# Five of a group's twenty fp32 sums, and two later adds, go from VectorE to GpSimd in a Strassen MLP

## The chip, the cores and the metric

One Trainium2 chip, one core of it. The metric is the device time of the whole program in microseconds; the traces are of one execution each.

## The reference

All in fp32. An attention without softmax (`out = q (k^T v)`, RMS-normalised) gives x of 8 x 576 tokens by 512 features. Then two MLPs with residuals follow, both 512 to 2048 to 512:

```python
# first: Fourier mixing and a norm ahead of the MLP
mixed = np.real(np.fft.fft(np.fft.fft(x, axis=1), axis=2))
u = x + mixed
un = (u - mean(u)) / np.sqrt(var(u) + 1e-6)
x2 = u + np.maximum(un @ w_ch1, 0.0) @ w_ch2
# second: a rank-32 mixing over the tokens
u = x2 + (x2.transpose(0, 2, 1) @ U @ V).transpose(0, 2, 1)
out = u + np.maximum(u @ w_ch1b, 0.0) @ w_ch2b
```

## The kernel before

**Stages.** Up to about 265 us of the span the attention and the Fourier transforms run, a batch at a time. All the rest is the two MLPs. The 4608 tokens are worked off in 12 groups g of 768: groups 0 to 5 are the first MLP, groups 6 to 11 (`g >= NS`) the second, over the same tokens.

**Products.** Each matrix product of a group is one level of Strassen's scheme: seven block products instead of eight, on sums and differences of blocks. In the up half (512 to 2048) the moving operands are sums of blocks of the input `a_sb`, in the down half (2048 to 512) sums of blocks of the hidden layer `h_sb`. `SIDE` says which: product 1 takes block 11 + 22, product 4 takes 21 - 11, 3 takes 12 - 22, 7 takes 21 + 22, 6 takes 11 + 12, and products 2 and 5 take one block alone. The down half runs over the products in the order 2, 5, 1, 4, 3, 7, 6 and over four quarters k of the hidden layer each: 28 steps.

**Splitting.** A step needs its 128 x 768 operand as two fp32r parts. For a product with two blocks there are three instructions, on three tiles of a ring of five entries: the sum `t_raw` (VectorE, `raw_dn`, L1358), its rounded part `t_hi` (ScalarE, `hi_dn`, L1073), and the rest `t_lo` = `t_raw` - `t_hi` (VectorE, `lo_dn`, L1339). TensorE then runs 12 matmuls (hi x hi, lo x hi, hi x lo, twice two; L832 to L834 in the up half, L849 to L851 in the down half). In the up half it is GpSimd that makes the sums (`raw`, L1569).

**Order.** Every engine has its order written out by hand: loops over g and over 56 steps t (28 up, 28 down), in which an engine issues what stands at its t. Entry n of the down half is used by TensorE at t = n + 28; the sum is issued at t = n + 24, `t_hi` at n + 25, `t_lo` at n + 26. `t_raw` of n waits for two things: that TensorE is through with the entry five before it in the ring (`entry_room`: the step before loop step n + 24 has ended) and that the hidden blocks are final (`blocks_final`). An engine takes its instructions strictly in the order issued.

VectorE further reads the results of the down half out of PSUM (`read`: d5 at t = 36, d1 at t = 40, d7 at t = 52, d6 at t = 56; in groups 6 to 11 also d4 at t = 44 and d3 at t = 48, which ScalarE does in groups 0 to 5). In groups 6 to 11 `add_first` (L1411, VectorE, t = 46 and 50) adds what d1 has left in `ch_sb` to the input blocks 11 and 22; both wait for d1, and d7 and d6 wait for both (`v_ready`).

In groups 0 and 6, the first of each MLP, the weights come unsplit: GpSimd sums pairs of weight blocks (`sum_slot`, L1559, at t = 20 to 30 and 40, 42, 44, 46, each behind its DMA), ScalarE rounds them (L981) and VectorE makes the rest (`split_slot_lo`, L1271). GpSimd otherwise has the up-half sums (at t = 5, 12, 52, 54, 55) and, in groups 1 to 4, the sums of the second MLP's weights.

Of the kernel before, what the change touches and what calls it, by code (L numbers as in the profile page):

```python
# [23 lines left out]
NS = NTILE // 2  # L24
NG = 2 * NS
NCH = 2 * CH
# [82 lines left out]
def dve_count(g, name, k=0):  # L109
    return sum(len(dve_events(x)) for x in range(g)) + [e[1:] for e in dve_events(g)].index((name, k)) + 1  # L110
# [45 lines left out]
def in_load_at(g):  # L156

    t = in_at(g)[1] // 2 * 2
    return t, t + 2


def build_program(nc, k_main, k_rest, v_main, v_rest, q_t, g_norm, wr1a, wr2a, wr1b, wr2b, u_perm, v_perm,
# [3 lines left out]
    ALU = mybir.AluOpType  # L166
# [90 lines left out]
    def a_block(g, name):  # L257
        a, b = int(name[0]) - 1, int(name[1]) - 1
        return a_sb[g % 2 if g >= NS else 0][:, 2 * a:2 * a + 2, TILE * b:TILE * (b + 1)]
# [4 lines left out]
    def ch_block(name):  # L264
        a, b = int(name[0]) - 1, int(name[1]) - 1
        return ch_sb[:, 2 * a:2 * a + 2, TILE * b:TILE * (b + 1)]
# [10 lines left out]
    with ExitStack() as ctx:  # L277
# [85 lines left out]
        def raw_made(g, e):  # L363

            pool = dve = 0
            for x in range(NENT * g + e + 1):
                gx, ex = divmod(x, NENT)
                if ex < len(UP_ENTRIES):
                    pool += len(SIDE[UP_ENTRIES[ex]]) > 1
                else:  # L370
                    dve += len(SIDE[DN_STEPS[ex - len(UP_ENTRIES)][0]]) > 1
            return pool, dve

        def sides(g, e):
# [536 lines left out]
        def _(act):  # L911
# [151 lines left out]
            def hi_dn(g, n):  # L1063
                i, k = DN_STEPS[n]
                e = len(UP_ENTRIES) + n
                r = (NENT * g + e) % ENT_RING
                if len(SIDE[i]) == 1:
                    act.wait_ge(step, entry_room(g, e))
                    act.wait_ge(act_read, act_count(g, "r" + SIDE[i][0], k))
                    nc.scalar.activation(t_hi[r][:, :, :], h_block(SIDE[i][0], k), ACT.Copy).then_inc(hi_ready, 1)  # L1070
                else:
                    act.wait_ge(raw_dve, raw_made(g, e)[1])
                    nc.scalar.activation(t_hi[r][:, :, :], t_raw[r][:, :, :], ACT.Copy).then_inc(hi_ready, 1)  # L1073

            def read(g, name, k):
# [120 lines left out]
        def _(dve):  # L1196
# [152 lines left out]

            def raw_dn(g, n):  # L1350
                i, k = DN_STEPS[n]
                if len(SIDE[i]) == 1:
                    return
                e = len(UP_ENTRIES) + n
                dve.wait_ge(step, entry_room(g, e))
                dve.wait_ge(act_read, blocks_final(g, e))
                x, y, op = sides(g, e)
                nc.vector.tensor_tensor(t_raw[(NENT * g + e) % ENT_RING][:, :, :], x, y, op).then_inc(raw_dve, 1)  # L1358

            def read(g, name, k):  # L1360
# [34 lines left out]
                else:  # L1395
# [8 lines left out]
                        if g > NS:  # L1404
                            dve.wait_ge(out_stored[block], 16 * (g - NS))
                    nc.vector.tensor_tensor(ch_block(block), both(DN_PAIR[i]), added, ALU.add).then_inc(dve_read, 1)

            def add_first(g, block):

                dve.wait_ge(dve_read, dve_count(g, "d1"))  # L1410
                nc.vector.tensor_tensor(a_block(g, block), a_block(g, block), ch_block("22"), ALU.add).then_inc(v_ready, 1)  # L1411

            def add_residual(g, j):
                n = NCH * g + j
# [31 lines left out]
            for g in range(NG):  # L1446
                more = g < NG - 1
                for t in range(NSTEP):
                    if g and t == 0:
                        read(g - 1, "d6", 0)  # L1450
                    if t == 0:
                        lo_up(g, 2)
                    if t == 2:
                        lo_up(g, 3)
                    if t == 3:
                        lo_up(g, 4)
                    for at, name, k in dve_events(g):
                        if at == t:
                            read(g, name, k)
                    if t == 8:  # L1460
                        lo_up(g, 5)
                    if t == 15:
                        lo_up(g, 6)
                    if t in (21, 22, 27, 28):
                        lo_dn(g, (21, 22, 27, 28).index(t))
                    if 29 <= t < 33:
                        lo_dn(g, t - 25)
                    if 34 <= t < 54:
                        lo_dn(g, t - 26)
                    if 32 <= t < 52:  # L1470
                        raw_dn(g, t - 24)
                    if g >= NS and t == 46:
                        add_first(g, "11")
                    if g >= NS and t == 50:
                        add_first(g, "22")
                    if more and t == 54:
                        lo_up(g + 1, 0)
                    if more and t == 55:
                        lo_up(g + 1, 1)
                    if g == 0 and t == 2:  # L1480
                        fix_row(B - 1)
                    if g == 0 and t == 36:
                        nc.vector.memset(up_raw[:, :, :], 0.0).then_inc(up_zeroed, 1)
                    if g == 0 and t == 43:
                        dve.wait_ge(up_split_hi, 1)
                        nc.vector.tensor_tensor(up_lo[:, :, :], up_raw[:, :, :], up_hi[:, :, :].bitcast(F32),
                                                ALU.subtract).then_inc(up_split_lo, 1)
                    if g == NS - 1 and t == 0:
                        dve.wait_ge(p_stored["v"], 32 * 8)
                        nc.vector.memset(vp_raw[:, :, :], 0.0).then_inc(vp_zeroed, 1)  # L1490
                    if g == NS - 1 and t == 9:
                        dve.wait_ge(vp_split_hi, 1)
                        nc.vector.tensor_tensor(vp_lo[:, :, :], vp_raw[:, :, :], vp_hi[:, :, :].bitcast(F32),
                                                ALU.subtract).then_inc(vp_split_lo, 1)
                    if 1 <= g <= NS:
                        if t - 1 in OUT_AT:
                            add_residual(g - 1, OUT_AT.index(t - 1))
                        if t - 3 in OUT_AT:
                            split_x2_lo(g - 1, OUT_AT.index(t - 3))
                        for P in range(4):  # L1500
                            n = 9 * P + 8
                            if n // NCH == g - 1 and t - 2 == GATHER_AT[n % NCH]:
                                turn_gathered(P)
                    if more:
                        if g + 1 < NS:
                            if t in LN_AT:
                                statistics(3 * (g + 1) + LN_AT.index(t))
                            if t - 2 in LN_AT:
                                layer_norm(3 * (g + 1) + LN_AT.index(t - 2))
                        elif t - 1 in mix_at(g):  # L1510
                            add_mixed(NCH * (g + 1) + mix_at(g).index(t - 1))
                    if (g, t - 8) in UNIT_AT:
                        split_unit_lo(UNIT_AT[g, t - 8])
                    for n in RAW_SLOTS:
                        if NSTEP * g + t == max(0, 2 * n - 6):
                            split_slot_lo(n)
# [3 lines left out]
        def _(pool):  # L1520
# [39 lines left out]

            def raw(g, e):
                r = (NENT * g + e) % ENT_RING
                pool.wait_ge(a_ready, NCH * (g + 1))
                if entry_room(g, e):
                    pool.wait_ge(step, entry_room(g, e))
                else:
                    stored_before(pool, e)
                x, y, op = sides(g, e)
                nc.gpsimd.tensor_tensor(t_raw[r][:, :, :], x, y, op).then_inc(raw_pool, 1)  # L1569

            for g in range(NT):
                weigh(0, g)
# [17 lines left out]
            for g in range(NG):  # L1590
                more = g < NG - 1
                for t in range(NSTEP):
                    if t == 5:
                        raw(g, 5)
                    if t == 12:
                        raw(g, 6)
                    if more and t == 52:
                        raw(g + 1, 0)
                    if more and t == 54:
                        raw(g + 1, 2)  # L1600
                    if more and t == 55:
                        raw(g + 1, 3)
                    if (g, t - 4) in UNIT_AT:
                        sum_unit(UNIT_AT[g, t - 4])
                    for n in RAW_SLOTS:
                        if NSTEP * g + t == 2 * n - 8 and summed_slot(n):
                            sum_slot(n)
# [74 lines left out]
```

## Time and profile before

| | us |
|---|---|
| median of 3 runs | 1824.33 |
| lowest and highest | 1823.0, 1835.87 |
| the profiled execution | 1823.0 |
| its span | 1820.9 |

The times are of the whole program; the span is that of the profiled execution's trace, from its first instruction to its last, and every row below counts from the span's start. PE is TensorE, DVE VectorE, ACT ScalarE, POOL GpSimd. An instruction's duration in the trace holds the time that it stood still for a memory port, so the same instruction with longer and shorter durations tells of something beside it. VectorE's instructions overlap by about 0.08 us, since one starts before the one ahead is written out.

### The profile page before, as it was taken

How to read it: one execution, taken by the hardware profiler on the slowest of the kernel's cores; microseconds unless marked ns; L12 is line 12 of the kernel's file. 1: busy time of each engine (PE TensorE's matmuls, PEld its weight loads, DVE VectorE, ACT ScalarE, POOL GpSimd, SP SyncE). 2: the span in 40 equal slices, each digit the busy share in tenths (PEclk: the TensorE clock that was granted, in tenths of full speed). 3: DMA queues.
4: the chain of work that ended last, by engine and by line, in shares of the span. 5: the costliest groups of instructions: out<-in, count | busy, mean ns of one | idle time of the engine just before them, and what ended most of it. 6: DMA issues, size and time to landing. Idle time of an engine off the chain costs nothing.

```text
span 1820.9 us, 25843 instructions
## 1 busy us (share of the span) xinstructions
PE 1738.5 (95%) x9908; PEld 1673.3 (92%) x9908; DVE 1374.4 (75%) x1631; ACT 786.0 (43%) x1126; POOL 432.9 (24%) x356
## 2 busy tenths in 40 slices
PE   6889879989999999999999999899999999999999
PEld 5667769979999999999999999799999999999999
DVE  5779987997777877867866858965956857758567
ACT  2333344554444544445444436434334434444442
POOL 2889973331120120120110013220110100100200
PEclk9889989999999999999999999999999999999999
DMA  8487557988787887887876778876766766767663
GB/s 256 161 272 250 201 201 282 370 332 283 262 303 261 283 287 258 289 286 247 297 260 232 257 246 310 333 275 231 251 236 237 257 234 242 255 231 254 224 249 128
DMA packets 123820, 470.04 MB, mean 258 GB/s; under 512 B 12274, under 2 KB 49650, under 8 KB 84019
## 3 DMA queue, kind: packets, MB, share of 16 engines
q1 hardware_dynamic: 122482, 467.21, 73.4%
q8 instruction: 81, 1.33, 0.3%
q10 hardware_dynamic: 1216, 1.18, 0.2%
q14 instruction: 41, 0.33, 0.0%
HBM read 389.70 MB, written 78.64 MB: 257 GB/s over the span
## 4 chain that ended last, share of the span: by engine, by line
PE 80%; DVE 12%; issue 3%; POOL 3%; DMA 2%; SPq 1%; ACT 0%; DVEq 0%; POOLq 0%; ACTq 0%
PE pair L832 12%; PE pair L834 12%; PE pair L833 12%; PE pair L849 12%; PE pair L851 12%; PE pair L850 12%; DVE t_lo L1339 2%; PE tr_ps L716 2%; PE pair L623 2%; DVE t_raw L1358 2%; DMA in_sb<-x_dram 1%; DVE w_sb L1271 1%; DMA v_sb<-v_rest 1%; DVE eo_sb L1229 1%; POOL x_sb L1528 1%
## 5 line engine op out<-in xcount | busy, mean ns | idle before, releaser
L849 PE MATMUL pair<-t_hi,w_sb 128*128 128x384 f32 x1344 | 460.4, 343 | 17.1 <-DVE t_lo L1339 16.7
L832 PE MATMUL pair<-t_hi,w_sb 128*128 128x384 f32 x1344 | 459.8, 342 | 7.0 <-DVE h_sb L1376 6.9
L851 PE MATMUL pair<-t_hi,w_sb 128*128 128x384 f32 x1344 | 456.9, 340 | 0.0
L850 PE MATMUL pair<-t_lo,w_sb 128*128 128x384 f32 x1344 | 456.8, 340 | 0.0
L833 PE MATMUL pair<-t_lo,w_sb 128*128 128x384 f32 x1344 | 455.1, 339 | 0.0
L834 PE MATMUL pair<-t_hi,w_sb 128*128 128x384 f32 x1344 | 455.0, 339 | 0.0
L1569 POOL TENSOR_TENSOR t_raw<-a_sb 128x768 f32<-128x768 f32 x60 | 126.1, 2103 | 920.1 <-PE pair L851 636.6
L1073 ACT ACTIVATE t_hi<-t_raw 128x768 fp32r<-128x768 f32 x240 | 202.6, 847 | 287.6 <-DVE t_raw L1358 287.6
L1339 DVE TENSOR_TENSOR t_lo<-t_raw,t_hi 128x768 fp32r<-128x768 f32 x300 | 306.7, 1028 | 12.9 <-ACT t_hi L1061 9.2
L849 PEld LDWEIGHTS pair<-t_hi,w_sb 128*128 128x128 f32 x1344 | 253.5, 189 | 23.8 <-DVE t_lo L1339 23.6
L832 PEld LDWEIGHTS pair<-t_hi,w_sb 128*128 128x128 f32 x1344 | 252.2, 188 | 14.3 <-issue 9.0
L1358 DVE TENSOR_TENSOR t_raw<-h_sb 128x768 f32<-128x768 f32 x240 | 241.1, 1005 | 23.4 <-PE pair L851 22.9
L833 PEld LDWEIGHTS pair<-t_lo,w_sb 128*128 128x128 f32 x1344 | 252.4, 188 | 3.1
L850 PEld LDWEIGHTS pair<-t_lo,w_sb 128*128 128x128 f32 x1344 | 253.6, 189 | 0.3
L851 PEld LDWEIGHTS pair<-t_hi,w_sb 128*128 128x128 f32 x1344 | 253.4, 189 | 0.0
L834 PEld LDWEIGHTS pair<-t_hi,w_sb 128*128 128x128 f32 x1344 | 252.2, 188 | 0.0
L1339 DVE TENSOR_TENSOR t_lo<-h_sb,t_hi 128x768 fp32r<-128x768 f32 x96 | 98.5, 1038 | 23.4 <-ACT t_hi L1070 23.4
L1380 DVE TENSOR_TENSOR h_sb<-pair,h_sb 128x768 f32<-128x768 f32 x48 | 46.0, 958 | 84.3 <-PE pair L834 84.2
L1271 DVE TENSOR_TENSOR w_sb<-w_raw,w_sb 128x1024 fp32r<-128x1024 f32 x76 | 105.1, 1383 | 2.4 <-ACT w_sb L981 2.3
L1528 POOL TENSOR_TENSOR x_sb<-x_sb,gn_sb 96x256 f32<-96x256 f32 x96 | 84.2, 908 | 57.7 <-DVE x_sb L1213 57.4
L1371 DVE TENSOR_TENSOR h_sb<-pair,h_sb 128x768 f32<-128x768 f32 x48 | 46.0, 958 | 65.9 <-PE pair L834 65.9
L1070 ACT ACTIVATE t_hi<-h_sb 128x768 fp32r<-128x768 f32 x96 | 78.7, 842 | 36.0 <-PE pair L851 32.6
(148 smaller groups left out, 2005.3 us busy)
## 6 DMA issues: line engine op xcount, KB each, us to landing
w_sb<-wc SPq DMA_DIRECT2D x260, 1024.0 KB, 4.9
wc<-w_sb SPq DMA_DIRECT2D x28, 1024.0 KB, 5.7
w_raw<-wr1a SPq DMA_DIRECT2D x24, 512.0 KB, 5.1
w_raw<-wr1b SPq DMA_DIRECT2D x24, 512.0 KB, 4.3
wc<-pb SPq DMA_DIRECT2D x16, 640.0 KB, 4.8
w_raw<-wr2a SPq DMA_DIRECT2D x10, 1024.0 KB, 7.0
wc<-pb_v SPq DMA_DIRECT2D x16, 640.0 KB, 5.7
w_raw<-wr2b SPq DMA_DIRECT2D x10, 1024.0 KB, 7.2
```

Source lines behind the costliest of these rows:

```text
L832: nc.tensor.matmul(ps, w_hi, hi[:, x, :], start=(fresh and x == 0), stop=False, skip_group_check=True)
L833: nc.tensor.matmul(ps, w_hi, lo[:, x, :], start=False, stop=False, skip_group_check=True)
L834: last = nc.tensor.matmul(ps, w_lo, hi[:, x, :], start=False, stop=(x == 1), skip_group_check=True)
L849: nc.tensor.matmul(ps, w_hi, hi[:, f, :], start=(fresh and k == 0 and f == 0), stop=False, skip_group_check=True)
L850: nc.tensor.matmul(ps, w_hi, lo[:, f, :], start=False, stop=False, skip_group_check=True)
L851: last = nc.tensor.matmul(ps, w_lo, hi[:, f, :], start=False, stop=(k == 3 and f == 1), skip_group_check=True)
L1073: nc.scalar.activation(t_hi[r][:, :, :], t_raw[r][:, :, :], ACT.Copy).then_inc(hi_ready, 1)
L1271: nc.vector.tensor_tensor(w_sb[r][:, 1, :, :, :], w_raw[r][:, 1, :, :, :], w_sb[r][:, 0, :, :, :].bitcast(F32), ALU.subtract).then_inc(w_l ...
L1339: nc.vector.tensor_tensor(t_lo[r][:, :, :], src, t_hi[r][:, :, :].bitcast(F32), ALU.subtract).then_inc(lo_ready, 1)
L1358: nc.vector.tensor_tensor(t_raw[(NENT * g + e) % ENT_RING][:, :, :], x, y, op).then_inc(raw_dve, 1)
L1528: last = nc.gpsimd.tensor_tensor(x, x, gn_sb[:, :].unsqueeze(1).to_broadcast([PT, H // 2, HD]), ALU.mult)
L1569: nc.gpsimd.tensor_tensor(t_raw[r][:, :, :], x, y, op).then_inc(raw_pool, 1)
```

## The change

The sum `t_raw` of every down-half entry with k = 3 is made by GpSimd instead of VectorE, where it is a sum of two blocks (products 1, 4, 3, 7, 6; loop steps t = 35, 39, 43, 47, 51). ScalarE waits for GpSimd's counter for these. Both `add_first` of groups 6 to 11 go to GpSimd too, to t = 41, behind each other. Within a loop step GpSimd issues the new instructions ahead of a weight sum of the same step. Nothing is left out or computed otherwise.

```diff
+POOL_KS = (3,)
+
+
+def by_pool(i, k):
+    return k in POOL_KS
@@ raw_made
-                    dve += len(SIDE[DN_STEPS[ex - len(UP_ENTRIES)][0]]) > 1
+                    i, k = DN_STEPS[ex - len(UP_ENTRIES)]
+                    if len(SIDE[i]) > 1:
+                        pool, dve = (pool + 1, dve) if by_pool(i, k) else (pool, dve + 1)
@@ scalar: hi_dn
-                    act.wait_ge(raw_dve, raw_made(g, e)[1])
+                    if by_pool(i, k):
+                        act.wait_ge(raw_pool, raw_made(g, e)[0])
+                    else:
+                        act.wait_ge(raw_dve, raw_made(g, e)[1])
@@ vector: raw_dn
-                if len(SIDE[i]) == 1:
+                if len(SIDE[i]) == 1 or by_pool(i, k):
                     return
@@ vector: add_first and its two calls
-            def add_first(g, block):
-
-                dve.wait_ge(dve_read, dve_count(g, "d1"))
-                nc.vector.tensor_tensor(a_block(g, block), a_block(g, block), ch_block("22"), ALU.add).then_inc(v_ready, 1)
...
-                    if g >= NS and t == 46:
-                        add_first(g, "11")
-                    if g >= NS and t == 50:
-                        add_first(g, "22")
@@ gpsimd: raw
-                pool.wait_ge(a_ready, NCH * (g + 1))
-                if entry_room(g, e):
+                if e < len(UP_ENTRIES):
+                    pool.wait_ge(a_ready, NCH * (g + 1))
+                    if entry_room(g, e):
+                        pool.wait_ge(step, entry_room(g, e))
+                    else:
+                        stored_before(pool, e)
+                else:
                     pool.wait_ge(step, entry_room(g, e))
-                else:
-                    stored_before(pool, e)
+                    pool.wait_ge(act_read, blocks_final(g, e))
                 x, y, op = sides(g, e)
                 nc.gpsimd.tensor_tensor(t_raw[r][:, :, :], x, y, op).then_inc(raw_pool, 1)
+
+            def raw_dn(g, n):
+                i, k = DN_STEPS[n]
+                if len(SIDE[i]) > 1 and by_pool(i, k):
+                    raw(g, len(UP_ENTRIES) + n)
+
+            def add_first(g, block):
+
+                pool.wait_ge(dve_read, dve_count(g, "d1"))
+                nc.gpsimd.tensor_tensor(a_block(g, block), a_block(g, block), ch_block("22"), ALU.add).then_inc(v_ready, 1)
@@ gpsimd: the loop over t
+                    if 32 <= t < 52:
+                        raw_dn(g, t - 24)
+                    if g >= NS and t == 41:
+                        add_first(g, "11")
+                        add_first(g, "22")
```

## Rows read from the trace of the kernel before

**Rows 1.** The page: its head, and busy time, share and instructions by engine.

```profile
span 1820.9 us, 25843 instructions
PE 1738.5 (95%) x9908; PEld 1673.3 (92%) x9908; DVE 1374.4 (75%) x1631; ACT 786.0 (43%) x1126; POOL 432.9 (24%) x356
```

**Rows 2.** Busy time of each engine in groups 0, 6 and 8.

```profile
core 0: us, PE busy (x) PEld busy (x) DVE busy (x) ACT busy (x) POOL busy (x), PEclk, DMA share, GB/s
285.00:404.00 119.00, 107.65 (x595) 103.88 (x594) 110.20 (x114) 60.92 (x77) 40.47 (x14) 0.99 0.93 345
...
1047.00:1191.00 144.00, 134.08 (x740) 128.21 (x740) 118.17 (x119) 69.30 (x87) 39.71 (x15) 0.98 0.84 303
...
1319.00:1445.00 126.00, 124.64 (x712) 123.63 (x711) 86.59 (x94) 52.86 (x66) 10.78 (x6) 1.00 0.70 242
```

**Rows 3.** TensorE's waits for `t_lo`: whole span, 280 to 410, 1080 to 1200.

```profile
PE pair L849 <- DVE t_lo L1339: 16.7, 16, 2.7
...
PE pair L849 <- DVE t_lo L1339: 8.6, 7, 2.2
...
PE pair L849 <- DVE t_lo L1339: 8.2, 9, 2.7
```

**Rows 4.** Busy time in finer stretches of groups 0, 6 and 8, columns as [rows 2].

```profile
355.00:395.00 40.00, 31.46 (x159) 28.90 (x158) 40.00 (x36) 17.86 (x22) 13.53 (x5) 0.96 0.92 336
1147.00:1197.00 50.00, 41.70 (x209) 38.08 (x208) 50.00 (x43) 20.20 (x24) 21.77 (x7) 0.93 0.88 328
1397.00:1437.00 40.00, 40.00 (x228) 40.00 (x228) 35.96 (x42) 15.79 (x19) 0.00 (x0) 1.00 0.75 253
```

**Rows 5.** Groups by line (busy, mean), and line L1569's durations (min/median/max, ns).

```profile
L1358 DVE TENSOR_TENSOR t_raw<-h_sb 128x768 f32<-128x768 f32 x240 | 241.1, 1005 | 23.4 <-PE pair L851 22.9
L1073 ACT ACTIVATE t_hi<-t_raw 128x768 fp32r<-128x768 f32 x240 | 202.6, 847 | 287.6 <-DVE t_raw L1358 287.6
...
L1569 POOL TENSOR_TENSOR t_raw<-a_sb x60: 1807/1855/4334, 260.0 to 1723.6; 128x768 f32<-128x768 f32 x60
```

**Rows 6.** Timeline of group 8: start, duration; VectorE, and starts of TensorE's steps.

```profile
1413.10 0.96 DVE L1388 TENSOR_TENSOR ch_sb<-pair,ch_sb 128x768 f32<-128x768 f32 x1 [0.57 <-PE pair L851]
1413.97 0.95 DVE L1339 TENSOR_TENSOR t_lo<-t_raw,t_hi 128x768 fp32r<-128x768 f32 x1
1414.84 0.95 DVE L1358 TENSOR_TENSOR t_raw<-h_sb 128x768 f32<-128x768 f32 x1
...
1417.45 0.95 DVE L1339 TENSOR_TENSOR t_lo<-t_raw,t_hi 128x768 fp32r<-128x768 f32 x1
...
1420.05 0.95 DVE L1358 TENSOR_TENSOR t_raw<-h_sb 128x768 f32<-128x768 f32 x1
1421.58 0.96 DVE L1394 TENSOR_TENSOR ch_sb<-pair,a_sb 128x768 f32<-128x768 f32 x1 [0.57 <-PE pair L851]
...
1419.26 0.34 PE L849 MATMUL pair<-t_hi,w_sb 128*128 128x384 f32 x1
...
1421.38 0.34 PE L849 MATMUL pair<-t_hi,w_sb 128*128 128x384 f32 x1
```

**Rows 7.** Timeline where GpSimd and VectorE run side by side: groups 8 and 0.

```profile
1438.65 2.10 POOL L1569 TENSOR_TENSOR t_raw<-a_sb 128x768 f32<-128x768 f32 x1 [86.11 <-PE pair L851]
1438.96 0.95 DVE L1406 TENSOR_TENSOR ch_sb<-pair,a_sb 128x768 f32<-128x768 f32 x1
1439.83 1.74 DVE L1339 TENSOR_TENSOR t_lo<-t_raw,t_hi 128x768 fp32r<-128x768 f32 x1
...
1442.89 2.12 POOL L1569 TENSOR_TENSOR t_raw<-a_sb 128x768 f32<-128x768 f32 x1 [2.14 <-PE pair L851]
1443.23 2.60 DVE L1339 TENSOR_TENSOR t_lo<-a_sb,t_hi 128x768 fp32r<-128x768 f32 x1
...
332.80 6.29 POOL L1559 TENSOR_TENSOR w_raw<-w_raw 128x1024 f32<-128x1024 f32 x1 [4.78 <-DMA w_raw<-wr2a]
...
361.42 2.75 POOL L1559 TENSOR_TENSOR w_raw<-w_raw 128x1024 f32<-128x1024 f32 x1 [2.90 <-DMA w_raw<-wr2a]
361.87 3.12 DVE L1358 TENSOR_TENSOR t_raw<-h_sb 128x768 f32<-128x768 f32 x1
```

## The prediction

> **What bounds the kernel now.** I read the page first: TensorE is busy for 95% of the span, VectorE for 75%, GpSimd for 24% [rows 1]. That looks like a kernel bound by TensorE with a VectorE in reserve, but a share over the whole span hides stages. So the windows by group came next [rows 2]: group 8 is an ordinary one, TensorE is full and VectorE has 39 of 126 us left, while groups 0 and 6 (where weights are still being summed and split) have VectorE at 110 of 119 and 118 of 144 us, and TensorE short. The waits of TensorE [rows 3] name one wait of the second phase that matters: 16.7 us for `t_lo` of L1339, 16 times. All 16 lie in groups 0 and 6. The finer windows [rows 4] show how much that is in all. In 40 undisturbed us of group 8 TensorE starts 228 matmuls, one every 0.175 us; in 355 to 395 us it starts 159, so 69 x 0.175 = 12 us are lost; in the 50 us from 1147 it starts 209 where 285 fit, 13 us lost. In both stretches VectorE is busy for every microsecond. The granted clock is 0.96 and 0.93 there and 1.00 in group 8. So some 25 us hang on VectorE's queue, and the rest of the second phase hangs on TensorE.
>
> **What is removed.** Five `t_raw` of each group (the last quarter, k = 3, of products 1, 4, 3, 7, 6) leave VectorE: 60 in all; in groups 6 to 11 the two `add_first` leave too: 12. Back to back, VectorE starts such an instruction every 0.87 us (1413.97, 1414.84 [rows 6]). So VectorE is freed of 60 x 0.87 + 12 x 0.87 = 63 us. In the ordinary groups this is worth nothing by itself, since TensorE doesn't wait for VectorE there. In groups 0 and 6 it would be 5 x 0.87 = 4.4 and 7 x 0.87 = 6.1 us.
>
> **What is added.** The same 72 instructions on GpSimd. VectorE's `t_raw` is 1.00 us on average; the nearest rows on GpSimd are its own `t_raw` of the same size, 1.86 us in the median of 60, up to 4.33 [rows 5]. 72 x 1.85 = 133 us more on an engine busy for 433 of 1821: there is room. The price is elsewhere. What happens when both engines work on SBUF is in [rows 7]. In group 8 GpSimd's `t_raw` starts at 1438.65; VectorE's L1406, which reads PSUM and one SBUF operand, takes its usual 0.95 us beside it; the `t_lo` after it, with two SBUF operands, takes 1.74 instead of 0.95. The `t_lo` at 1443.23 behind another GpSimd `t_raw` takes 2.60, and the `t_raw` at 361.87 behind a GpSimd weight sum 3.12. The excess ends each time with the GpSimd instruction: VectorE doesn't slow down, it stands still. The other way round GpSimd stands still too: its weight sum at 332.80 took 6.29 us, the same one at 361.42 only 2.75.
>
> So a moved instruction gives VectorE 0.87 and takes back 0.79 (1.74 - 0.95, when a PSUM read covers half of it) to 1.65 (2.60 - 0.95): net -0.08 to +0.78 us for each, if VectorE is busy at the time; nothing if GpSimd falls into a gap. The Trainium skill (SBUF — State Buffer, "Who interferes with whom") says the same of a VectorE instruction with two SBUF inputs and a GpSimd one that reads SBUF: whichever gets the pair first holds it for the whole instruction, the other blocks fully. By that rule alone, every one of the 72 meeting a busy VectorE would cost the upper figure; the trace agrees on the standing still, but shows GpSimd also passed over (6.29 us), which is what gives the lower figure.
>
> **Where the moved ones fall.** The raw at loop step t may start when step t-1 has ended. They are at t = 35, 39, 43, 47, 51, and VectorE's next item is always a read of PSUM at t+1 (36, 40, 44, 48, 52; in groups 0 to 5 those of 44 and 48 are ScalarE's). In group 8 VectorE has a gap there: it waits 0.57 us for the read at 1413.10 and for that at 1421.58 [rows 6], 1.4 us once the raw before is gone. GpSimd's 1.85 us then lies in the gap and under the PSUM read. So the 35, 39, 47, 51 of the ordinary groups cost nothing. For the `t_lo` that follows, GpSimd has two loop steps of time (12 x 0.175 = 2.1 us each) against 1.85 + 0.85 on ScalarE [rows 5]: no wait. If that cover is gone, it costs 0.78 each.
>
> *Groups 7 to 11, the adds.* They are the dear part. Both wait for d1, whose sum ends at 1414.05, and stand in GpSimd's queue ahead of the raw of t = 43. VectorE works without a pause from 1413.10 to 1421.00 here. If GpSimd gets in after each VectorE instruction, the two adds and the raw (allowed at 1419.26, the start of step 43) block three VectorE instructions, 3 x 1.65 = 4.95 us, before the `t_lo` that ends at 1417.45 + 0.95 = 1418.40. TensorE needs that at 1421.38 (step 44): 2.98 us to spare, so it waits 2.0 us. If GpSimd is held off until the gap after 1420, the adds run at about 1420.1 and 1422.0, the raw of 43 ends near 1426.4, ScalarE's part and the `t_lo` near 1428.2, and step 47 (start 1421.38 + 3 x 2.12 = 1427.7) waits 0.5. A wait costs more than itself: 25 us were lost for 16.7 us of waits in 16, of which some 5 are half clock (0.04 x 40 + 0.07 x 50), so 0.2 us each; say 0.3. That is 0.8 to 2.3 us for each of five groups, 4 to 11.5. Both orders occur in [rows 7], so I take the middle, 7.5.
>
> *Group 0.* VectorE has no gap. Five raws x (-0.08 to +0.78) = -0.4 to 3.9 us. GpSimd gets in at once as often as not, and the sums in its queue make alternation likelier; I take 2.5. The raw of t = 43 stands behind the sum of t = 42, which waits for its weights' DMA ([rows 7]: 2.90 us idle before 361.42); it is still needed only two loop steps later by a VectorE that is late itself, so no price.
>
> *Group 6.* Seven x (-0.08 to +0.78) = -0.6 to 5.5 us. The adds stand between the weight sums here; three GpSimd instructions more in a stretch where the sums already block; I take 4.5.
>
> *Clock.* A longer stall can lengthen the half-clock stretch that it brings, now 0.07 x 50 = 3.5 us in group 6: 0 to 5 us, I take 1.5. *Groups 1 to 5* have no adds and, as group 8, no wait for `t_lo` [rows 3]; should one blocked `t_lo` become late there, that is 0.78 + 0.3, so 0 to 1 us; I take 0.
>
> Sum: 7.5 + 2.5 + 4.5 + 1.5 = 16 us on the profiled execution's own 1823.0 us (span 1820.9 plus 2.1 around it), which is 1.3 below the median shown: **1839 us**. Bounds from the ends: 4 - 0.4 - 0.6 = +3 to 11.5 + 3.9 + 5.5 + 5 + 1 = +27.
>
> **Rivals.** *Relief* (the other side, if too little for the 1%): in groups 0 and 6 GpSimd slips its work wholly under PSUM reads and waits, VectorE is 10.5 us shorter there and TensorE follows, and the adds find gaps: 1823 - 10.5 = 1812. For it: VectorE is the cause of the 25 us. Against: in groups 0 and 6 there is no gap to slip into [rows 4]. It decides once the mean block of a moved instruction is below the 0.87 us that moving it frees. *Nothing moves*: GpSimd is held off and gets in only under PSUM reads, -0.08 each, the adds cost the lower end: 1823 + 3 = 1826. For it: the 6.29 us sum. *Full alternation*: every moved instruction blocks 1.65 and stalls bring clock: 1823 + 27 = 1850, with some more if groups 1 to 5 begin to stall as well.
>
> **How the numbers follow.** Forecast 0.50, nothing moves 0.17, full alternation 0.22, relief 0.11. Range: 1816 to 1855. A measurement of this kernel tells about 1% from no change, 18 us: faster than 1806 needs more than relief gives: 0.04. Slower than 1842.6 holds the rival of full alternation and the upper third of the forecast: 0.36. Within 1%: 0.60.
>
> **What would show it.** `t_lo` and `t_raw` of VectorE get a longer mean though there are 60 fewer of them; GpSimd's `t_raw` and `add_first` show 2.1 to 2.6 us, some over 4. TensorE's wait for `t_lo` rises above 16.7 us and has new entries in groups 7 to 11, one or two a group near steps 44 to 47. Wrong would be: no wait there (the adds found room), or fewer than 12 and 13 us lost in groups 0 and 6 (relief), or a wait for GpSimd on ScalarE that reaches TensorE (then the queue order, not the blocking, sets the price).

## The result and the profile after

| | before | changed |
|---|---|---|
| median, 8 runs each, us | 1832.2 | 1849.01 |
| lowest and highest | 1823.0, 1835.87 | 1840.04, 1852.56 |
| the profiled execution | 1823.0 | 1847.24 |
| its span | 1820.9 | 1844.9 |

The ratio is 1.0101, with an interval of 1.0079 to 1.0124: the changed kernel is slower by about 18.5 us. The ratio rests on more runs than the table's eight (25 of the changed kernel, with a median of 1849.86), whose medians alone are 16.8 us apart. The two profiled executions are 24.2 us apart. Single executions differ by more than the effect: in the twelve traces of this case group 0 begins between 263.6 and 278.6 us, though no kernel changes anything ahead of it. So amounts for a whole kernel go by ratios, and amounts of a stretch by the lengths of the groups below.

The page of the changed kernel, its head, the engines and the groups by line (busy, mean in ns, idle time before them and its releaser); the last line is of the full list of groups:

```profile
span 1844.9 us, 25843 instructions
PE 1744.3 (95%) x9908; PEld 1677.4 (91%) x9908; DVE 1376.6 (75%) x1559; ACT 784.6 (43%) x1126; POOL 612.4 (33%) x428
...
L1351 DVE TENSOR_TENSOR t_lo<-t_raw,t_hi 128x768 fp32r<-128x768 f32 x300 | 345.4, 1158 | 13.5 <-ACT t_hi L1070 10.0
L1576 POOL TENSOR_TENSOR t_raw<-h_sb 128x768 f32<-128x768 f32 x60 | 152.0, 2534 | 575.5 <-PE pair L860 575.5
...
L1370 DVE TENSOR_TENSOR t_raw<-h_sb 128x768 f32<-128x768 f32 x180 | 207.6, 1154 | 19.8 <-PE pair L860 19.8
...
L1586 POOL TENSOR_TENSOR a_sb<-a_sb,ch_sb 128x768 f32<-128x768 f32 x12 | 30.0, 2522 | 5.6 <-DVE ch_sb L1400 5.6
```

VectorE executes 72 instructions fewer than in [rows 1] (1559 against 1631) and is busy 2.2 us longer (1376.6 against 1374.4). The 63 us that were to be freed are all there again, as longer durations: its `t_raw` takes 1154 ns on average instead of the 1005 of [rows 5]. The 60 moved sums take GpSimd 2.53 us each and the 12 moved adds 2.52, where the prediction had 1.85 for the instruction alone. The busy share of VectorE, 75% on both pages, tells nothing of this; instructions and means do.

TensorE's waits for `t_lo` in the changed kernel: whole span, group 0 (280 to 414 us), group 6 with its neighbours (1060 to 1215), and the rest (1215 to 1845). The columns are the sum in us, the number, and the longest:

```profile
PE pair L858 <- DVE t_lo L1351: 34.2, 24, 5.5
...
PE pair L858 <- DVE t_lo L1351: 12.5, 7, 3.4
...
PE pair L858 <- DVE t_lo L1351: 13.7, 7, 5.5
...
PE pair L858 <- DVE t_lo L1351: 8.0, 10, 1.0
```

Against [rows 3] the waits of groups 0 and 6 grew from 8.6 and 8.2 to 12.5 and 13.7, and the last line is new: ten waits in groups 7 to 11, two of them in group 8.

How long each group takes, from its first matmul to the next group's (in us, from the traces; "t32" is the part of groups 0 and 6 from step 32 on, in which all moved instructions lie; g7-10 is a mean of four; e1 to e10 are the experiments below; groups 1 to 3 take 129.0 to 129.2 in all of them but e9, where they take 133.7, and group 5 takes 130.9 in all):

```
                           g0     g0 t32  g4     g6     g6 t32  g7-10  g11
before                     137.3  63.6    129.1  146.5  66.4    125.6  118.8
changed                    145.1  68.3    129.4  150.8  71.1    127.7  120.9
e1 sums only               143.3  64.7    129.5  147.4  67.4    125.7  118.8
e2 adds only               141.6  63.5    129.0  147.2  67.2    126.5  119.6
e3 adds at t = 46, 50      141.0  64.6    129.4  150.5  70.5    128.5  119.2
e4 late weight sums, DVE   134.3  60.3    129.1  143.1  63.0    125.6  118.8
e5 idle adds               138.3  63.8    129.1  145.9  66.3    129.1  120.3
e6 idle fills              137.6  63.2    129.1  145.6  65.8    125.8  118.8
e7 sums, not in g0, g6     136.9  63.2    129.4  148.1  66.3    125.7  118.8
e8 all weight sums, DVE    134.4  61.3    129.0  145.3  64.3    125.7  118.8
e9 two quarters            144.7  71.1    133.6  153.6  73.9    130.4  121.5
e10 changed, e4's edit     137.8  63.0    129.5  146.8  66.8    127.8  120.9
```

Where nothing in them differs, groups 1 to 5 and 7 to 11 repeat to 0.3 us, so one trace is enough to read them. Groups 0 and 6 do not: group 0 took 136.9, 137.3, 137.6, 138.3 and 141.6 in the five traces in which nothing in it differs. But that spread lies ahead of t = 32: from there on the same five took 63.2 to 63.8, and group 6 took 65.8 to 66.4 in the four in which nothing in it differs. So for these two groups the columns t32 are the ones to compare. In the changed kernel's group 0, 3.1 of the 7.8 us more were lost before t = 32, ahead of any moved sum, and 4.7 behind it.

### The profile page after: what moved, and what is told of

The parts are those of the page before. It is cut to its first block, busy times and chain, and to the rows that moved or that the text cites. A ratio compares the mean times of both kernels' runs of the same rounds, so it can differ in the third digit from the quotient of the medians.

```text
span 1844.9 us, 25843 instructions
## 1 busy us (share of the span) xinstructions
PE 1744.3 (95%) x9908; PEld 1677.4 (91%) x9908; DVE 1376.6 (75%) x1559; ACT 784.6 (43%) x1126; POOL 612.4 (33%) x428
## 4 chain that ended last, share of the span: by engine, by line
PE 75%; DVE 12%; issue 4%; POOL 4%; DMA 3%; ACT 1%; SPq 1%; DVEq 0%; POOLq 0%; ACTq 0%
PE pair L841 11%; PE pair L843 11%; PE pair L842 11%; PE pair L858 11%; PE pair L860 11%; PE pair L859 11%; DVE t_raw L1370 2%; DVE t_lo L1351 2%; PE tr_ps L725 2%; PE pair L632 2%; DMA in_sb<-x_dram 1%; PE pair L653 1%; DVE w_sb L1283 1%; POOL t_raw L1576 1%; DVE eo_sb L1241 1%
## 5 line engine op out<-in xcount | busy, mean ns | idle before, releaser
L1351 DVE TENSOR_TENSOR t_lo<-t_raw,t_hi 128x768 fp32r<-128x768 f32 x300 | 345.4, 1158 | 13.5 <-ACT t_hi L1070 10.0
L1576 POOL TENSOR_TENSOR t_raw<-h_sb 128x768 f32<-128x768 f32 x60 | 152.0, 2534 | 575.5 <-PE pair L860 575.5
L1370 DVE TENSOR_TENSOR t_raw<-h_sb 128x768 f32<-128x768 f32 x180 | 207.6, 1154 | 19.8 <-PE pair L860 19.8
L1283 DVE TENSOR_TENSOR w_sb<-w_raw,w_sb 128x1024 fp32r<-128x1024 f32 x76 | 109.9, 1446 | 4.3 <-ACT w_sb L990 4.3
L1351 DVE TENSOR_TENSOR t_lo<-h_sb,t_hi 128x768 fp32r<-128x768 f32 x96 | 93.8, 989 | 23.4 <-ACT t_hi L1079 23.4
L1383 DVE TENSOR_TENSOR h_sb<-pair,h_sb 128x768 f32<-128x768 f32 x48 | 46.0, 958 | 65.8 <-PE pair L843 65.8
```

Source lines behind the costliest of these rows:

```text
L1283: nc.vector.tensor_tensor(w_sb[r][:, 1, :, :, :], w_raw[r][:, 1, :, :, :], w_sb[r][:, 0, :, :, :].bitcast(F32), ALU.subtract).then_inc(w_l ...
L1351: nc.vector.tensor_tensor(t_lo[r][:, :, :], src, t_hi[r][:, :, :].bitcast(F32), ALU.subtract).then_inc(lo_ready, 1)
```

## The experiments

The numbers in the expectations are against the kernel before, unless they say otherwise. Theory, as it stood on both traces: every GpSimd instruction that reads SBUF blocks a whole VectorE instruction with two SBUF operands, and the time is lost where a `t_lo` has less slack than the blocks that pile up ahead of it. Rival: GpSimd's longer queue (late sums, weight sums held up behind the new instructions) sets the price.

### e1 and e2: each half of the change alone

e1 keeps the moved sums and takes the adds back to VectorE:

```diff
@@ vector, t = 46 and 50
+                    if g >= NS and t == 46:
+                        add_first(g, "11")
+                    if g >= NS and t == 50:
+                        add_first(g, "22")
@@ gpsimd, t = 41
-                        add_first(g, "11")
-                        add_first(g, "22")
```

> The five sums a group (k = 3) are on GpSimd as in the changed kernel; both adds are back on VectorE at t = 46 and 50. Theory (GpSimd and VectorE exclude each other; only pile-ups behind which TensorE has no slack cost time): groups 7 to 11 keep their old length of 125.7 us, since each sum falls in the gap ahead of a PSUM read, so 10 us of the changed kernel's loss are gone; groups 0 and 6 keep theirs, some 4 to 8 us together: 0.2 to 0.5% slower than before. Rival (the sums are dear wherever they are, by their longer chain over GpSimd): groups 7 to 11 still have 127.7 us each and the whole is 0.8% slower or more.

Measured: 1834.67 against 1828.0, ratio 1.0045 (1.0026 to 1.0063), 8.2 us. Groups 7 to 11 are as before to 0.1 us. The one trace shows less than the ratio: from t = 32 on groups 0 and 6 are 1.0 us longer each, and all groups together, leaving out what comes before t = 32 in these two, less than 3 us, below the 4.8 us at which the interval of the ratio begins.

e2 keeps the moved adds and takes the sums back:

```diff
-POOL_KS = (3,)
+POOL_KS = ()
```

> Only the two adds of groups 6 to 11 are on GpSimd at t = 41; all sums stay on VectorE. Theory: in groups 7 to 11 two blocks of 1.65 us meet 2.98 us of slack at step 44, so TensorE waits 0.3 us where it waited 1.7 to 2.0 with the third block by the sum of t = 43: 0.3 to 0.6 us a group, group 0 unchanged, group 6 0 to 3 us longer: 0.1 to 0.3% slower. Rival (the adds alone carry the 2.1 us a group): groups 7 to 11 at 127.7 us, 0.6% slower or more.

Measured: 1832.72, ratio 1.0023 (1.001 to 1.0036), 4.2 us, and 0.85 a group in groups 7 to 11 (5 x 0.85 = 4.2). That is above the 0.3 to 0.6 expected: two adds block 2 x 1.65 = 3.3 us ahead of the `t_lo` of step 43, which had 2.6 us to spare where the expectation counted with the 2.98 of step 44, and TensorE starts step 43 0.76 us late.

The halves give 8.2 + 4.2 = 12.4 of 18.5 us. The rest is their product: in groups 7 to 11 adds alone cost 0.85 a group, sums alone 0.1, both together 2.1, since the sum of t = 43 is then a third block, ahead of the `t_lo` of step 44. Group 6 from t = 32 on shows the same: 1.0 for the sums, 0.8 for the adds, 4.7 for both.

### e7: the sums, but not in groups 0 and 6

```diff
-def by_pool(i, k):
-    return k in POOL_KS
+def by_pool(g, i, k):
+    return k in POOL_KS and g % NS > 0
@@ the adds back on VectorE, as in e1
```

> The five sums a group go to GpSimd in groups 1 to 5 and 7 to 11 only, 50 in all; in groups 0 and 6 and for the adds all is as before. Theory (a GpSimd sum is free where VectorE has gaps or TensorE has slack): same as before within 0.1%, at most 0.4 us in group 4. Rival: the 0.45% of all sums on GpSimd is spread evenly, so 50 of 60 still cost 0.35% or more.

Measured: 1826.81 against 1828.82, ratio 0.9995 (0.997 to 1.002). 50 sums moved in ordinary groups cost nothing that can be measured; so e1's 8.2 us (4.8 to 11.5 by its interval) would come mostly or wholly from the ten sums of groups 0 and 6, about 0.8 us for each. In the traces the five sums of group 0 cost 1.0 us in e1 and in e3 and 4.7 in the changed kernel, with the same instructions each time. So a moved sum costs something there, between 0.2 and 0.9 us, and no run fixes it closer.

### e5 and e6: is it the reading, or the queue?

Both leave the kernel before as it is and add GpSimd instructions on a tile that nobody uses, at the changed kernel's places (two at t = 41 behind d1, one at t = 43). In e5 they are additions, in e6 fills, which write the same tile and read nothing:

```diff
+                    if g > NS and t == 30:
+                        extra(g, t)
+                    if g > NS and t == 41:
+                        extra(g, t)
+                        extra(g, t)
+                    if g > NS and t == 43:
+                        extra(g, t)
@@ extra, at t = 41 and 43 (at t = 30 a fill in both)
+                # e5
+                nc.gpsimd.tensor_tensor(idle_sb, idle_sb, idle_sb, ALU.add)
+                # e6
+                nc.gpsimd.memset(idle_sb, 0.0)
```

> The kernel before with all its work where it was, and in groups 7 to 11 three extra fp32 additions on GpSimd over a tile of 128x768 that nothing else reads: two at t = 41 behind d1, one at t = 43 (a fill of the tile at t = 30 too). No engine waits for them. Theory (exclusion alone makes the loss): each stops VectorE for 1.65 us, VectorE is freed of nothing, and TensorE loses 2.0 to 2.5 us at steps 42 to 44 of each of these groups: 127.7 to 128.2 us instead of 125.7; group 11 alike. Rival (the loss comes from waiting for GpSimd's late results, its queue or its latency): nobody waits for these results, so the groups stay at 125.7.

> As the run with idle additions, but the extra GpSimd instructions only fill the tile (they write 128x768 and read nothing). Theory (it is the reading of SBUF on both sides that excludes): VectorE's instructions beside them keep 0.95 us and the groups 125.7 us. Rival (any GpSimd access to SBUF stops VectorE): instructions beside a fill are longer by up to its duration.

Measured, one execution each: e5 1847.99, e6 1833.32, beside a median of 1828.82 before. What counts is group 7 to 9: 128.4 us in e5 (2.8 above before), 125.8 or less in e6. (Group 10 of e5 took 131.2, with a half-clock stretch of 3.4 us in it: TensorE's granted clock was at its lower level, 1.2 GHz.) The timeline of group 8 (start, duration, both in us) in e5:

```profile
1427.31 2.23 DVE L1360 TENSOR_TENSOR t_raw<-h_sb 128x768 f32<-128x768 f32 x1
1429.45 2.22 DVE L1341 TENSOR_TENSOR t_lo<-t_raw,t_hi 128x768 fp32r<-128x768 f32 x1
...
1426.60 4.25 POOL L1586 TENSOR_TENSOR idle_sb<-idle_sb 128x768 f32<-128x768 f32 x2 [21.47 <-DVE ch_sb L1390]
```

and in e6:

```profile
1423.99 0.95 DVE L1341 TENSOR_TENSOR t_lo<-t_raw,t_hi 128x768 fp32r<-128x768 f32 x1
1424.85 0.95 DVE L1360 TENSOR_TENSOR t_raw<-h_sb 128x768 f32<-128x768 f32 x1
1425.72 0.95 DVE L1341 TENSOR_TENSOR t_lo<-t_raw,t_hi 128x768 fp32r<-128x768 f32 x1
...
1424.13 1.60 POOL L1586 MEMSET idle_sb<- 128x768 f32 x2 [21.45 <-DVE ch_sb L1390]
```

Nothing waits for these instructions, so no data arrives late and no sum is delayed by a queue; yet e5 alone reproduces the loss of groups 7 to 9, and a bit more than the 127.7 to 128.2 expected; that VectorE keeps its own sums and adds would explain it, but wasn't tested. Fills beside the same VectorE instructions leave each at 0.95. A fill is also shorter (0.80 us against 2.1), so e6 alone would leave duration as an explanation; but VectorE's three instructions beside the fills show no lengthening at all. For groups 7 to 11 this settles it against the queue: the price is what GpSimd's additions do to VectorE's instructions. What an addition has and a fill lacks is the reading of SBUF, so by these two runs it is the reading, not the writing, that collides.

### e3: the adds on GpSimd, but apart

```diff
@@ gpsimd
-                    if g >= NS and t == 41:
-                        add_first(g, "11")
-                        add_first(g, "22")
+                    if g >= NS and t == 46:
+                        add_first(g, "11")
+                    if g >= NS and t == 50:
+                        add_first(g, "22")
```

> The changed kernel with its two adds still on GpSimd, but at t = 46 and t = 50, where VectorE had them. Theory (it is three GpSimd instructions in a row behind d1 that cost): apart, each blocks 1.65 us against at least 2 us of slack, groups 7 to 11 are back at 125.7 us, and 4 to 8 us of groups 0 and 6 stay: 0.2 to 0.5% slower than before. Rival (what VectorE stands still in all decides): the same number of instructions blocks the same time, groups 7 to 11 stay near 127.7 us and the whole at 1% slower.

Measured: 1854.99, ratio 1.0154 (1.0105 to 1.0203): not faster than the changed kernel (1.0101), as the theory had it. Whether it is slower isn't clear, since the intervals overlap. The timeline of group 8 shows what the expectation had overlooked (GpSimd's rows, two of VectorE's, and the TensorE step that waits):

```profile
1440.11 2.33 POOL L1576 TENSOR_TENSOR t_raw<-h_sb 128x768 f32<-128x768 f32 x1 [6.15 <-PE pair L860]
1442.41 1.85 POOL L1586 TENSOR_TENSOR a_sb<-a_sb,ch_sb 128x768 f32<-128x768 f32 x1
1448.59 2.54 POOL L1576 TENSOR_TENSOR t_raw<-h_sb 128x768 f32<-128x768 f32 x1 [4.33 <-PE pair L860]
1451.08 2.58 POOL L1586 TENSOR_TENSOR a_sb<-a_sb,ch_sb 128x768 f32<-128x768 f32 x1
1457.07 2.57 POOL L1576 TENSOR_TENSOR t_raw<-h_sb 128x768 f32<-128x768 f32 x1 [3.41 <-PE pair L860]
1459.60 2.54 POOL L1576 TENSOR_TENSOR t_raw<-a_sb 128x768 f32<-128x768 f32 x1
...
1457.87 2.59 DVE L1370 TENSOR_TENSOR t_raw<-h_sb 128x768 f32<-128x768 f32 x1
1460.38 2.58 DVE L1351 TENSOR_TENSOR t_lo<-t_raw,t_hi 128x768 fp32r<-128x768 f32 x1
...
1463.02 0.44 PE L858 MATMUL pair<-t_hi,w_sb 128*128 128x384 f32 x1 [1.79 <-DVE t_lo L1351]
```

A loop step fixes only the order in the queue. d1 is long done at t = 46, so each add runs directly behind the sum ahead of it: two pairs of blocks instead of one triple, and they lie late in the stretch, just ahead of the sums of t = 51 and 52. From its read of t = 44 to the `t_lo` of step 53 VectorE is blocked 1.06 + 1.65 + 0.80 + 1.65 + 1.65 = 6.8 us and freed of three instructions (both adds and the sum of t = 47), 2.6 us; the `t_lo` of step 53 had 2.3 us to spare before. 2.3 + 2.6 - 6.8 = -1.9, and TensorE waits 1.79. So the quantity that decides is the sum of blocks since VectorE last ran ahead, less what it was freed of, against the slack of the step. In the trace groups 7 to 11 are 12 us longer than before, 3.2 of them with half-clock stretches of 3.4 us in groups 9 and 10 (129.3 us each against 127.7 in 7 and 8); from t = 32 on group 6 is 4.1 us longer and group 0 1.0. That is 17 of the ratio's 28 us (19 to 37 by its interval, over four runs); the other 11 are open.

### e9: a second quarter of the sums on GpSimd

```diff
 def by_pool(i, k):
-    return k in POOL_KS
+    return k in (1, 3)
@@ the adds back on VectorE, as in e1
```

> As the run with the five sums a group on GpSimd and the adds on VectorE (0.45% slower than before), but with the sums of k = 1 there too: ten a group, 120 in all. Theory (each costs its block less the 0.87 us freed where VectorE has no gap): groups 0 and 6 lose twice the 8 us; group 4, where the slack is already used up, 1 us; groups 7 to 11 had 0.3 to 0.7 us left near steps 53 and 54, and lose up to 1 us each: 17 to 24 us, 0.9 to 1.3% slower. Rival (freeing VectorE catches up once enough is moved, since it has 104 us less to do): not slower than the 0.45% of half as many.

Measured: 1893.46 against 1835.06, ratio 1.0314 (1.029 to 1.0339), 58 us, far above the 0.9 to 1.3% expected. Doubling the moved sums costs seven times e1's 8.2 us. Busy time of each engine in the last 40 us of group 2 and of group 5, both of the first MLP (columns as [rows 2]), in e9:

```profile
650.00:690.00 40.00, 37.34 (x204) 35.71 (x205) 39.28 (x29) 17.25 (x23) 21.52 (x10) 1.00 0.78 285
1048.30:1088.30 40.00, 40.00 (x229) 39.87 (x228) 39.96 (x29) 18.08 (x23) 23.82 (x11) 1.00 0.71 261
```

and in the last 40 us of group 2 and of group 5 of the kernel before:

```profile
620.00:660.00 40.00, 40.00 (x228) 40.00 (x227) 36.10 (x38) 19.28 (x23) 5.66 (x3) 1.00 0.88 310
1009.00:1049.00 40.00, 40.00 (x229) 39.87 (x229) 34.40 (x36) 17.86 (x22) 5.57 (x3) 1.00 0.74 262
```

In group 2 VectorE executes 29 instructions instead of 38 and is yet busy for 39.3 instead of 36.1 us (1.35 us for each instead of 0.95), and TensorE starts 204 matmuls instead of 228. Groups 1 to 4, where e7's single quarter was free (0.3 us in group 4), lose 4.6 us each, 0.9 us for each of the second five sums. Group 5 has ten moved sums too and loses nothing: it had less for VectorE to do before (34.4 us), and though VectorE is now busy for all of the 40 us, TensorE starts its 229 matmuls as before. So the price is convex: nothing while gaps and slack take the blocks, and then about what a block takes less what the move frees (0.78 us), or somewhat more.

### e4, e8 and e10: the other way round

If GpSimd's reading is dear in groups 0 and 6, it must pay to take reading off GpSimd there. e4 is the kernel before with the last four weight sums of groups 0 and 6 (slots 24 to 27, the late ones) on VectorE, rounding and rest one loop step later:

```diff
+def by_dve(n):
+    return n % NSLOT >= 24
@@ vector
+                        if NSTEP * g + t == 2 * n - 7 and summed_slot(n) and by_dve(n):
+                            sum_slot(n)      # on nc.vector
@@ gpsimd
-                        if NSTEP * g + t == 2 * n - 8 and summed_slot(n):
+                        if NSTEP * g + t == 2 * n - 8 and summed_slot(n) and not by_dve(n):
```

> The kernel before, with the last four weight sums of group 0 and of group 6 (slots 24 to 27) taken from GpSimd and given to VectorE, each one loop step later, and their two halves of the splitting a loop step later too. Theory (exclusion): VectorE does such a sum in about 1.15 us, and stands still 2.2 us for GpSimd's; each of the two groups gets 4 x 1.05 = 4 us shorter, with some half-clock time less, 6 to 12 us in all, 0.3 to 0.7% faster than before, though VectorE, the late engine there, gets 9 us more work. Rival (VectorE's own work decides): 9 us slower.

Measured: 1819.62 against 1828.0, ratio 0.9956 (0.9941 to 0.9972), 8 us faster. In the trace, the group of the moved sums, one of them in group 0, and TensorE's waits for `t_lo` over the whole span:

```profile
L1276 DVE TENSOR_TENSOR w_raw<-w_raw 128x1024 f32<-128x1024 f32 x8 | 9.7, 1214 | 0.0
...
363.40 1.22 DVE L1276 TENSOR_TENSOR w_raw<-w_raw 128x1024 f32<-128x1024 f32 x1
...
PE pair L853 <- DVE t_lo L1349: 11.3, 12, 2.5
```

The engine that was the bound of these groups got eight instructions of 1.21 us more, and the waits for it fell from 16.7 to 11.3 us. From t = 32 on both groups are 3.4 us shorter. A rival is that the weight sums merely come earlier. It doesn't hold: in the kernel before VectorE waits for nothing from 335 to 404 and from 1130 to 1197 us (the list of its waits is empty there), so sums that come earlier could not by themselves have made it faster; its own instructions had to get shorter. This version beats both kernels.

e8 gives VectorE all twenty weight sums (`by_dve` returns True):

> The kernel before with all 20 weight sums of groups 0 and 6 on VectorE, each one loop step later (the run with 8 of them there was 0.44% faster). Theory (exclusion): the twelve early ones stand in a stretch where VectorE still has gaps, so they give less: 0.5 to 0.8% faster than before, 0 to 6 us better than 8 alone. Rival (VectorE's total work in these groups now decides): 12 x 1.15 = 14 us more of it, slower than the run with 8, near the time of before.

Measured: 1822.66 against 1828.82, ratio 0.9966 (0.9946 to 0.9986). Not better than e4: the theory's further gain did not come. The early sums lie at t = 20 to 30; from t = 32 on groups 0 and 6 take 61.3 and 64.3 us against 60.3 and 63.0 in e4. Why the further sums give nothing, no run shows.

e10 is the changed kernel with e4's edit, so that no late weight sum stands in GpSimd's queue with the moved ones:

> The changed kernel with the last four weight sums of groups 0 and 6 on VectorE, which alone made the kernel before 0.44% faster. Theory: in groups 0 and 6 four blocks of 2.2 us go for 4 x 1.15 us of own work, as before, and groups 7 to 11 stay at 127.7 us: 0.4 to 0.65% slower than before. Rival (GpSimd's queue held by weight sums was what made the moved sums dear in groups 0 and 6): with the queue free these groups lose nothing more by the moved sums, and only the 10 us of groups 7 to 11 less 8 us are left: 0.1% slower.

Measured: 1846.62 against 1835.06, ratio 1.0056 (1.0023 to 1.0088). The gain over the changed kernel's 1.0101 is 0.45%, what e4's edit gave by itself (0.44%), though both intervals leave room for a difference of some 0.3%. Were the weight sums held up behind the moved instructions the main cause, freeing them would have given back more than it gives without the change. For a part the rival stays open: from t = 32 on the edit shortens groups 0 and 6 of the changed kernel by 5.3 and 4.3 us, and of the kernel before by 3.4 each, though single traces of the sums in group 0 differ by as much (e1, e3 and the changed kernel, above). A moved sum can be late without a weight sum in its queue: in group 0 of e10 the two sums from t = 43 on took GpSimd 12.73 us together, and VectorE then stood idle 2.61 us for the first. Groups 7 to 11 stay at 127.8 and 120.9.

## Why the prediction was right, and where it was short

The forecast was +16 us (a ratio of 1.0088), the measured ratio 1.0101 (+18.5 us), inside the range. The predicted 1839 lies 10 us under the changed kernel's median, of which 9.2 us are the base: the kernel before is 1832.2 in eight runs, not the 1823.0 of its profiled execution. The sign and the mechanism held; by the chances, though, "within 1%" had 0.60 and the ratio came out on its edge, 1.01% with an interval over both sides.

| term | forecast | the changed kernel's trace |
|---|---|---|
| groups 7 to 11 | 7.5 (0.8 to 2.3 a group) | 10.5 (2.1 a group) |
| group 0, from t = 32 on | 2.5 | 4.7 (1.0 in e1 and e3) |
| group 6, from t = 32 on | 4.5 | 4.7 |
| clock | 1.5 | within the two above |
| groups 1 to 5 | 0 (0 to 1) | 0.3 (group 4) |
| sum | 16 | 20.2; 18.5 by the ratio |

**The adds of groups 7 to 11, right but mis-sized.** The prediction had two orders and took their middle. The chip takes one of them, in all five groups: GpSimd gets in behind each VectorE instruction. The timeline of group 8 of the changed kernel, VectorE and then GpSimd:

```profile
1428.49 0.96 DVE L1400 TENSOR_TENSOR ch_sb<-pair,ch_sb 128x768 f32<-128x768 f32 x1 [1.44 <-PE pair L860]
1429.36 0.95 DVE L1351 TENSOR_TENSOR t_lo<-t_raw,t_hi 128x768 fp32r<-128x768 f32 x1
1430.23 2.60 DVE L1370 TENSOR_TENSOR t_raw<-h_sb 128x768 f32<-128x768 f32 x1
1432.75 2.60 DVE L1351 TENSOR_TENSOR t_lo<-t_raw,t_hi 128x768 fp32r<-128x768 f32 x1
1435.27 2.59 DVE L1370 TENSOR_TENSOR t_raw<-h_sb 128x768 f32<-128x768 f32 x1
1437.79 0.94 DVE L1351 TENSOR_TENSOR t_lo<-t_raw,t_hi 128x768 fp32r<-128x768 f32 x1
...
1429.53 5.01 POOL L1586 TENSOR_TENSOR a_sb<-a_sb,ch_sb 128x768 f32<-128x768 f32 x2 [0.77 <-DVE ch_sb L1400]
1434.89 2.16 POOL L1576 TENSOR_TENSOR t_raw<-h_sb 128x768 f32<-128x768 f32 x1 [0.36 <-PE pair L860]
```

The three 2.60s are the three blocks of 1.65 and the last `t_lo` is the one that the prediction had at 1418.40 in [rows 6]. The gap ahead of d1 is 1.44 us, as forecast from 0.57. Steps 42 and 43 then take 2.88 and 3.38 us instead of 2.12, together 2.0 us more, what the upper branch had for its wait. It comes in two parts, since two blocks already make the `t_lo` of step 43 late; TensorE's waits between 1400 and 1500 are these two:

```profile
PE pair L858 <- DVE t_lo L1351: 1.6, 2, 1.0
```

The failed part is the choice "both orders occur, so I take the middle": 7.5 us where the upper order alone gives 11.5 and 10.5 were measured. The Trainium skill's rule that the prediction weighed (SBUF — State Buffer, "Who interferes with whom") is what happened here: each blocked instruction stood still until the GpSimd one had ended, 2.60 us beside 0.95.

**The other sums of ordinary groups cost nothing.** The forecast holds: e7 and e1 leave groups 7 to 11 at 125.7 (before 125.6) and groups 1 to 4 within 0.4 us.

**Groups 0 and 6.** The changed kernel's trace has 4.7 + 4.7 = 9.4 us where the prediction had 2.5 + 4.5 + 1.5 = 8.5. That this is so near is partly luck: with the same instructions group 0 lost only 1.0 us in e1 and e3, so 2.5 is a right order of size and no more. In group 6 the adds are dear beside the sums (1.0 and 0.8 alone, 4.7 together), as the prediction's higher figure for it had it. Of the clock: from t = 32 on the kernel before has half-clock stretches (granted clock at the lower level of 1.2 GHz) of 3.4 us in group 0 and 6.8 in group 6, the changed kernel two of 3.4 in group 0 and 6.8 + 3.4 in group 6. One stretch of 3.4 us more in each is, by estimate, worth at most half its length, 1.7 us. (The 3.5 us that the prediction calls the stretch of group 6 is what the stretch of 6.8 us costs at half speed.) What stays unexplained is e1's ratio: 8.2 us for the sums alone, of which its trace shows less than 3.

**A late result of GpSimd in group 0: overlooked.** The prediction gave GpSimd's sum two loop steps, found them enough, and counted its being passed over as VectorE's gain (-0.08). The timeline of group 0 of the changed kernel, where GpSimd's row is the sum of t = 47:

```profile
388.00 7.43 POOL L1576 TENSOR_TENSOR t_raw<-h_sb 128x768 f32<-128x768 f32 x1 [6.98 <-PE pair L860]
391.65 0.95 DVE L1370 TENSOR_TENSOR t_raw<-h_sb 128x768 f32<-128x768 f32 x1
392.52 1.21 DVE L1283 TENSOR_TENSOR w_sb<-w_raw,w_sb 128x1024 fp32r<-128x1024 f32 x1
...
395.46 1.58 ACT L1085 ACTIVATE t_hi<-t_raw 128x768 fp32r<-128x768 f32 x2 [4.08 <-POOL t_raw L1576]
396.34 0.96 DVE L1351 TENSOR_TENSOR t_lo<-t_raw,t_hi 128x768 fp32r<-128x768 f32 x1 [2.61 <-ACT t_hi L1085]
397.22 2.59 DVE L1370 TENSOR_TENSOR t_raw<-h_sb 128x768 f32<-128x768 f32 x1
```

The instruction is held off for 7.43 - 1.85 = 5.6 us by VectorE's back-to-back ones. Its result is needed; ScalarE waits 4.08 us, then VectorE, the engine whose queue sets this group, stands idle 2.61 us. After that its next two sums are blocked (397.22 above) with no slack left, and TensorE's steps 50 to 52 take 3.3 us more than before. In groups 0 to 5 ScalarE does the PSUM read of t = 48, so VectorE has no such read there under which GpSimd could get in; that this is the reason is argued, not shown. This is the last thing named in the prediction as what would make it wrong, and it did occur, once in this trace and once in e10's, but not in e1's or e3's; and the queue is not the price in groups 7 to 11 (e5), nor the main one in groups 0 and 6 by the ratios (e10).

**The rivals.** Relief falls: e1 is slower, not faster, with VectorE freed of 60 x 0.87 us. "Nothing moves" falls with the new waits in groups 7 to 11. Full alternation (1850, +27) describes the order in groups 7 to 11 rightly; that the median of 1849 lies beside its 1850 comes of the base, since +27 is not the +18.5 of the ratio. Without its 5 us of clock and its 1 us for groups 1 to 5 it has 11.5 + 3.9 + 5.5 = 20.9, near the 20.2 of the trace: it had the order right and the clock too dear.

## What to carry to other kernels

Moving elementwise work with two SBUF operands from a partly idle VectorE to an idle GpSimd frees 0.87 us and can cost 1.65 of the same VectorE; count each moved instruction against the slack of the next result that someone waits for, adding the blocks since VectorE's last gap, and the cost is nothing below that slack and whole above it. Where VectorE is the bound, the opposite move can pay: GpSimd's weight sums, put on the overloaded VectorE, made the kernel 0.44% faster. A place in the program of an engine is a place in its queue, not a time. And where whole executions differ by more than the effect, compare the stretch that the change touches, and look first how well it repeats where nothing differs.

## What the runs showed of the hardware

- Who is passed over is lopsided by circumstance: beside back-to-back VectorE instructions with two SBUF operands, GpSimd gets in after one of them (1429.53 above) or is held off for 5.6 us (388.00 above); in e10 two such sums took 12.73 us together. What decides between the two, no run here shows.
- Additions collide, fills don't, as expected for e5 and e6: two fills of 128 x 768 took 1.60 us beside VectorE instructions that kept their 0.95 us (e6), two additions of the same size took 4.25 us and lengthened VectorE's to 2.23 (e5).
- Giving the overloaded engine more work made TensorE wait less for it: in e4 a weight sum took VectorE 1.21 us, while the same sum on GpSimd had taken 2.75 us [rows 7] and stopped a VectorE `t_raw` for 3.12 - 0.95 = 2.2 us.
